# Gram products of head pairs on 64-row halves of the TensorE array, without the zero-padded key copy

## The reference, cut to what matters

```python
def _attn_ref(q, k, v, beta):            # B=4 batches, H=8 heads, S=768, D=48
    k_n = k / (np.linalg.norm(k, axis=-1, keepdims=True) + 1e-06)
    for t in range(S):
        y[:, :, t] = einsum('bhd,bhde->bhe', q[:, :, t], state)
        v_old = einsum('bhde,bhd->bhe', state, k_n[:, :, t])
        state += beta[:, :, t] * outer(k_n[:, :, t], v[:, :, t] - v_old)
    return y
...
x = _moe_ref(attn_out, U, V, w_ch1, w_ch2)     # mixing over the sequence, then two 384x1536 products
return _moe2_ref(x, w_ch1, w_ch2)              # real part of a 2-D FFT, layer norm, two 384x1536 products
```

## Time and profile before

| | us |
|---|---|
| runs | 1260.3, 1266.56, 1274.25 |
| median | 1266.56 |
| the profiled execution, first to last instruction | 1268.3 |
| attention, up to the last state product (L695), its start | 514.2 |
| PE busy over the span | 1173.2 |
| DVE busy | 590.1 |
| ACT busy | 449.0 |
| mean granted clock of TensorE | 0.968 |

### The profile page before, as it was taken

How to read it: one execution, slowest core, us unless ns; L and a number is a source line. 1 busy time by engine, 2 the same in 40 slices (tenths; PEclk the granted TensorE clock), 3 DMA queues, 4 the chain that set the end, 5 groups by cost and what they waited for, 6 DMA issues and landing times. The chain is left out here.

```text
span 1268.3 us, 24886 instructions
## 1 busy us (share of the span) xinstructions
PE 1173.2 (93%) x9978; PEld 1118.7 (88%) x9978; DVE 590.1 (47%) x1116; ACT 449.0 (35%) x853; POOL 116.1 (9%) x117
## 2 busy tenths in 40 slices
PE   4699999998999999599999999996799999999998
PEld 3598888888889888499999999995799999999998
DVE  7557776567764673352222222324553433434322
ACT  2566666565665653141211111212231221221211
POOL 4112211122111210000000000000000000000000
PEclk9899999999998997699999999998899999999999
DMA  5111112212112110441010100001111001001001
GB/s 98 26 32 34 31 26 37 39 26 39 22 33 39 51 62 29 127 151 52 1 38 1 37 0 0 1 1 52 48 52 38 19 1 38 19 0 37 19 16 40
DMA packets 98535, 44.87 MB, mean 35 GB/s; under 512 B 78037, under 2 KB 97162, under 8 KB 98314
## 3 DMA queue, kind: packets, MB, share of 16 engines
q1 hardware_dynamic: 98442, 43.47, 13.4%
HBM read 34.03 MB, written 11.85 MB: 36 GB/s over the span
## 5 line engine op out<-in xcount | busy, mean ns | idle before, releaser
L1220 DVE SCALAR_TENSOR_TENSOR hid_l_mix<-up_mix,hid_h_mix 128x384 fp32r<-128x384 f32 x96 | 53.4, 557 | 209.2 <-ACT hid_h_mix L1165 209.2
L382 DVE CAST_PREDICATED zi<-merge_mask,zb 128x512 f16<-128x512 uint8 x144 | 100.5, 699 | 98.8 <-PE zb L630 97.9
L1220 DVE SCALAR_TENSOR_TENSOR hid_l_dft<-up_dft,hid_h_dft 128x384 fp32r<-128x384 f32 x96 | 53.5, 557 | 183.9 <-ACT hid_h_dft L1165 183.8
L1165 ACT ACTIVATE hid_h_dft<-up_dft 128x384 fp32r<-128x384 f32 x96 | 47.2, 492 | 255.8 <-PE up_dft L1330 255.8
L1165 ACT ACTIVATE hid_h_mix<-up_mix 128x384 fp32r<-128x384 f32 x96 | 47.2, 492 | 245.7 <-PE up_mix L1330 245.7
L525 ACT CAST xi<-xb 128x512 f16<-128x512 f32 x144 | 82.3, 590 | 110.5 <-PE xb L656 68.8
L733 PE MATMUL pb<-kq_t,kz 128*128 128x256 f32 x384 | 99.2, 404 | 4.3 <-DVE nr L423 4.2
L1328 PE MATMUL dn_mix<-w2h_mix,hid_h_mix 128*128 128x384 f32 x288 | 99.5, 346 | 3.0 <-DVE hid_l_mix L1220 2.5
L1328 PE MATMUL dn_dft<-w2h_dft,hid_h_dft 128*128 128x384 f32 x288 | 98.5, 342 | 0.1
L1328 PE MATMUL up_mix<-act_h_mix,w1h_mix 128*128 128x384 f32 x288 | 97.1, 337 | 1.2 <-DVE act_l_mix L1238 1.2
L1328 PE MATMUL up_dft<-act_h_dft,w1h_dft 128*128 128x384 f32 x288 | 97.0, 337 | 1.2 <-DVE act_l_dft L1238 1.2
(11 more groups left out here) (170 smaller groups left out, 2476.8 us busy)
## 6 DMA issues: line engine op xcount, KB each, us to landing
k_raw<-k SPq DMA_DIRECT2D x24, 192.0 KB, 3.3
q_raw<-q SPq DMA_DIRECT2D x24, 192.0 KB, 3.5
v_in<-v SPq DMA_DIRECT2D x24, 192.0 KB, 3.2
stage_mix<-moe_w_ch SPq DMA_DIRECT2D x12, 384.0 KB, 4.5
stage_dft<-moe_w_ch SPq DMA_DIRECT2D x12, 384.0 KB, 3.8
x_rows<-x_sb SPq DMA_DIRECT2D x6, 384.0 KB
x_now_mix<-x_sb SPq DMA_DIRECT2D x4, 576.0 KB, 3.9
x_now_mix<-x_mem SPq DMA_DIRECT2D x4, 576.0 KB, 5.0
```

The lines of the kernel that those rows point to most:

```text
L382: nc.vector.copy_predicated(blocks_all(zi[:, lv - 1, g], 1 << lv, 1), merge_mask[:, lv - 1].rearrange("p (n b) -> p n b", b=1 << lv), zb[g ...
L1165: nc.scalar.activation(hid_h[:, f % 2], up_b[f % 2][:, 0:HALF], ACT.Relu).then_inc(s_hh, 1)
L1220: nc.vector.scalar_tensor_tensor(hid_l[:, f % 2], up_b[f % 2][:, 0:HALF], 0.0, hid_h[:, f % 2], ALU.max, ALU.subtract).then_inc(s_hl, 1)
```

## The change

The diff drops `kz`, with its clearing on POOL and the two ACT copies that filled it. A gram product now reads its keys from `kq_t` itself: 64 partitions, 0 to 63 for an even head and 64 to 127 for an odd one, both as the stationary and as the moving operand. Even heads write pb[0] and odd heads pb[1], alternating, so that two products that stand next to each other use different halves of the rows of the array and different banks. The waits change too: one wait ahead of all four products, for both banks.

```diff
--- before.py
+++ after.py
@@ -136,7 +136,6 @@
     v_in = sb("v_in", [C, B, H, D], F32)
     norms = sb("norms", [C, 2, 2 * H], F32)
     kn = sb("kn", [C, 2, H, DP], F32)
-    kz = sb("kz", [C, 2, H, C], F32)
     n_h = sb("n_h", [C, 2, H, C], F16)
     kb = sb("kb", [C, B, H, DP], F32)
     kq_t = sb("kq_t", [C, B, HP, 2, C], F32)
@@ -298,7 +297,7 @@
                         pool.wait_ge(s_kb, pp)
                     nc.gpsimd.tensor_tensor(kn[:], k_raw[:], k_raw[:], ALU.mult).then_inc(s_sq, 1)
                     if isinstance(s, int) and s == -2:
-                        for t in (kz, x0, w_f):
+                        for t in (x0, w_f):
                             nc.gpsimd.memset(t[:], 0.0).then_inc(s_pads, 1)
 
                 def unsolved(g):
@@ -419,7 +418,7 @@
                     for n in range(2):
                         dve.wait_ge(s_pfull, PU * pp + 4 + 4 * g + 2 * j + n + 1)
                         for u in range(2):
-                            h = 4 * j + 2 * n + u
+                            h = 4 * j + 2 * u + n
                             last = nc.vector.scalar_tensor_tensor(
                                 nr[:, 2 * par + g, h], pb[n][:, 256 * u:256 * u + 256],
                                 beta_now[:, par, g, h:h + 1], gram_mask[:], ALU.mult, ALU.mult)
@@ -540,14 +539,10 @@
                     if not prep:
                         return
                     if isinstance(s, int) and s == -2:
-                        act.wait_ge(s_pads, 5)
+                        act.wait_ge(s_pads, 4)
                     act.wait_ge(s_pfull, PU * pp + g + 1)
-                    src = pb[g][:].rearrange("p (a t) -> p a t", t=C)
-                    nc.scalar.copy(kq_t[:, 2 * par + g, :, 0], src)
-                    for o in range(2):
-                        half = slice(DP * o, DP * o + DP)
-                        last = nc.scalar.copy(kz[half, g].rearrange("p (a o) t -> p a o t", o=2)[:, :, o], src[half])
-                    last.then_inc(s_pkq, 1)
+                    nc.scalar.copy(kq_t[:, 2 * par + g, :, 0],
+                                   pb[g][:].rearrange("p (a t) -> p a t", t=C)).then_inc(s_pkq, 1)
 
                 def queries(g):
                     if not prep:
@@ -610,7 +605,7 @@
             for a in range(2):
                 nc.tensor.transpose(pb[a][:, 0:96], beta_rows[:, a], ident[0:96, 0:96]).then_inc(s_beta_ps, 1)
             pe.wait_ge(s_beta, 2)
-            pe.wait_ge(s_pads, 5)
+            pe.wait_ge(s_pads, 4)
 
             def body(s, par, it):
                 prep, inv, chain = active(s)
@@ -722,18 +717,18 @@
                 def gram(g, j):
                     if not prep:
                         return
-                    for n in range(2):
-
-                        if g == 0 and j == 0:
-                            pe.wait_ge(s_pkq, 4 * pp + 3 + n)
-                        else:
-                            pe.wait_ge(s_pgr, 8 * pp + 4 * g + 2 * j + n - 1)
-                        for u in range(2):
-                            h = 4 * j + 2 * n + u
-                            last = nc.tensor.matmul(pb[n][:, 256 * u:256 * u + 256], kz[:, g, h],
-                                                    kq_t[:, 2 * par + g, h // 2].rearrange("p a t -> p (a t)"),
-                                                    start=True, stop=True)
-                        last.then_inc(s_pfull, 1)
+                    if g == 0 and j == 0:
+                        pe.wait_ge(s_pkq, 4 * pp + 4)
+                    else:
+                        pe.wait_ge(s_pgr, 8 * pp + 4 * g + 2 * j)
+                    for u in range(2):
+                        for n in range(2):
+                            rows = slice(DP * n, DP * n + DP)
+                            pair = kq_t[rows, 2 * par + g, 2 * j + u]
+                            last = nc.tensor.matmul(pb[n][:, 256 * u:256 * u + 256], pair[:, 0],
+                                                    pair.rearrange("p a t -> p (a t)"), start=True, stop=True)
+                            if u == 1:
+                                last.then_inc(s_pfull, 1)
 
                 def turn_n(g):
                     if not prep:
```

## The result

The changed kernel is slower: 1.030 times the kernel before, 95% interval 1.023 to 1.038. Its four runs took 1297.03, 1311.4, 1314.77 and 1343.62 us (median 1313.09) beside 1269.66 for the kernel before. The forecast was 1291.5 with a range of 1280 to 1313: the direction and the wait behind it are right, the size is short by some 20 us, and the profile tells where those lie. That the median sits at the upper end of the range is luck: this end was rival (a)'s time, and the trace rules (a) out.

The account below looks back on a forecast made before the run. The prediction took a ring through DVE's last gram evictions to bound each slot; 2.30 us in each of ten slots, +0.55 and +1.4 in the bodies ahead made +25 us on 1266.56: 1291.5, range 1280 to 1313.

Parts of the forecast that it names:

- rival (a): Gram products: row halves don't run side by side, pb[0] fills 0.43 us later four times a slot; 1312 us, chance 0.12.
- the ring through DVE's last evictions: One slot: when the fourth gram piece's last eviction ends counts, then DVE's queue, state, `hop(1, 1)`, PE's 21 us, grams.
- Part 1: Gram products on half arrays: records run in four pairs, 0.95 us a piece in place of 1.81.
- Part 2: Gram banks: DVE gets its first full bank at +1.11 us as before, evictions still end at +2.89.
- Part 3: Between gram pieces: waiting for both banks puts them 2.95 us apart, not 2.28, 2.51 and 2.51; +1.55 us a slot.
- Part 4: Ahead of the first gram: it now waits for ACT's last query copy, out of pb[1], too; +0.75 us.
- Part 5: Dropping kz's two ACT copies a batch: 0 in full slots, -1.75 us in body(-1); its clearing on POOL 0.
- Who gets the delay: After the fourth gram everything follows DVE: the whole shift, +2.30 us, goes into the slot; PE's saving becomes idle time.
- Rival (c): Ahead of `hop(1, 1)`: PE's 1.65 us idle time absorbs the delay, no change; 1275 us, chance 0.05.
- body(-2): Body with preparation alone: gram pieces one at a time, two at half clock, last at full; +1.4 us.
- Rival (d): PE idle some 1.3 us in three gaps lowers the clock, some 3 us a slot; 1325 us, chance 0.04.
- The sum: Ten full slots 23.0 us, body(-1) +0.55, preparation-only body +1.4: in all +25 us on the 1266.56 median.

Follow-up runs that it names:

- the four-bank version: Changed kernel with gram pieces alternating between the two cb and the two pb banks, each waiting for the piece two before: 1245.9 to 1311.4 us, median 1273.6.

## Why the prediction was right, and where it was short

- **What bounds the kernel** (the ring through DVE's last evictions): right. Cutting PE's gram time from 1.81 to 1.07 us a piece gave nothing, and delaying the evictions went into the slot one to one.
- **Part 1, half arrays**: right in kind. The eight records stand in pairs, one row 1.13 us long. The next piece starts 1.07 us after the first record (322.15 to 323.22), where 0.95 and up to 0.11 for the mode change were taken. Rival (a), no overlap, is out, and with it the upper end of the range.
- **Part 2, banks full at the same time as before**: 1.17 against 1.15. The evictions themselves shrank by 0.08, which I had held constant.
- **Part 3, the joint wait**: 3 x 2.88 = 8.64 against 7.30, so +1.34 where +1.55 was forecast; shown, together with part 4, by putting the waits alone into the old kernel (+29.8 us) and by taking them out of the new one (no loss).
- **Part 4, the first wait**: 0.75, as read; but moving the copy gave only 0.15 back.
- **Part 5, kz**: 0 in the full slots and -1.75 in body(-1), both shown (39.95; 1.77).
- **Who gets the delay**: 1.34 + 0.75 - 0.08 = 2.01, the slot measured 39.94 - 37.95 = 1.99. Rival (c), absorption, is out: PE's wait for the state grew from 1.65 to 2.08 us.
- **body(-2)**: the last eviction came 2.25 us later (38.76 against 36.51), 1.4 was forecast; all three gaps ran at half the clock, I had taken the last at full.
- **The clock** is the step that failed. Rival (d) said: "The new idle times are shorter than either, so I think it stays", chance 0.04. It counted the three new gaps, which are, and left the old one ahead of `hop(1, 1)` at 1.65 us. That one grew to 2.08, longer than the 1.7 that it was compared with, as in every profile with a fourth piece of about 1 us. From body(0) to body(9), the loop's edge left aside, every fall in every profile came behind a wait of that length. I had also priced a fall at 3 us in every slot; it is 11.3 us in some slots and nothing in the others, two in the profiled run, 22.5 us in all.
- **The sum**: 25 forecast, 17.0 measured in the attention once the 22.5 are taken out. The slots gave 2.0 in place of 2.3, and the clock at the end of the attention, lower in the kernel before, took about 4 off. The feed-forward stages added 4.9 that no term was meant for.

## What to carry to other kernels

When a faster producer shares a pair of banks with a consumer that takes longer than it does, look at the order in which the banks become full and free, not at the producer's time: interleaving two banks makes both full late and both needed at once, which turns a double buffer into a single one. Before speeding up an engine that the next wait will stop anyway, find the buffer that would let it run ahead. And where an engine's clock depends on its work, price each idle time also by the clock behind it, the old ones with the new: work that gets shorter lengthens the wait behind it.

## What the hardware showed that I had not expected

- Two fp32 products of 64 rows each, on opposite halves and in opposite banks, run at the full pace of each: eight records in 1.13 us where eight whole-array records take 1.97.
- Once down, the clock stayed at 1.2 GHz for 23.9 us while PE worked without any pause (23.80 of 23.80 us busy). Each such stretch cost 11.3 us. At the loop's edge it was back after 3.4 or 6.8 us, and four times behind the wait of 2.08 after 3.4.
- The clock never fell behind waits of 0.35 to 1.72 us for the state update (45 of them), and behind 16 of 46 of 2.04 to 2.08 us.
- Behind useless products in an idle time of 2.08 us the runs of the changed kernel scatter by 7 us in place of 47, and those of the four-bank version by 17 in place of 66.
